# Unread products at the start, W1's raw copy in another place and its low parts on GpSimd, and a new order of the opening

## The chip, the cores and the metric

The kernel runs on one core of a Trainium2 chip. The metric is the device time of one execution in microseconds; a kernel's time is the median of its runs. Engines are named TensorE, VectorE, ScalarE, GpSimd and SyncE; in the rows they are PE (and PEld for its weight loads), DVE, ACT, POOL and SP, and a q behind a name is that engine's queue of transfers.

## What is computed

A linear attention with a decaying state, and two feed-forward stages behind it, all in float32. Batch 4, 8 heads, 768 tokens, head width 48; the model width is 8 x 48 = 384.

```python
for t in range(S):
    cur = einsum('bhd,bhe->bhde', u * k[t], v[t])
    y[t] = einsum('bhd,bhde->bhe', r[t], state + cur)
    state = w[t][..., None] * state + einsum('bhd,bhe->bhde', k[t], v[t])
h = y @ w_in                       # 3072 x 384 @ 384 x 1024
solu = h * softmax(h)
ln = (solu - mean(solu)) / sqrt(var(solu) + 1e-6) * g_ln
x2 = ln @ w_out                    # 1024 -> 384
g = maximum(0.01 * (x2 @ w_in2), x2 @ w_in2)     # 384 -> 2048
out = g @ w_out2                   # 2048 -> 384
```

## The kernel before

**Tiles.** The 768 tokens of each batch are cut into six chunks of 128. Three chunks make a super of 384 tokens. Attention and the first feed-forward stage up to the normalised rows go chunk by chunk; the matrix products behind them go super by super, 384 columns wide.

**A chunk.** Its decays are multiplied up by a scan (`decay`, L854), their inverse is taken (`inverse`, L864), the keys are divided by them (`undecayed_keys`, L869), GpSimd multiplies the queries by them (`decayed_queries`, L515) and ScalarE lays the queries of two heads side by side in `rb` (`part_heads`, L660). TensorE makes the scores (`scores`), VectorE masks them (`mask`, L877), GpSimd makes the keys as seen from the chunk's end (`end_keys`, L524), TensorE transposes these (`transpose_keys`, L1205) and ScalarE copies them out (`take_keys`, L682). `attend` makes the chunk's output, `fresh_state` its part of the state, `take_y` (L890) and `take_state` (L899 and L904) bring both back. ScalarE sums the decays and inverses for a later test of their range (`take_range`, L676). The output is transposed (`transpose_y`, L1198), copied to X (`take_x`, L667), multiplied with W1 (the expert product, 128 x 1024), its row maximum taken (`row_max`, L921), then the exponential (`exp_rows`, L643), the product with it (`times_exp`, L931), its statistics (`row_stats`, `row_moments`, L937 to L951), the row's scale on GpSimd (`row_scale`, L548 and L550) and the normalised rows (`normalise`, L650).

**Two ways of multiplying.** The steady part splits each weight and each moving operand into a high part, rounded to fp32r, and a low part, what is left, and uses three products (`HH`, `LH`, `HL`). ScalarE makes a weight's high part (`high_part`, L639) and VectorE the low one (`low_part`, L1014), both in groups of 768 columns: four for W1 and W2, eight for W3 and W4. The raw weight lies where the low part will be. The first three chunks can't wait for that, so they are multiplied in plain float32 out of the raw weights (two records in the trace for each product). For this reason `low_part(0, g)` waits until all six halves of the first expert products are done (`pe_h`), since it writes over what they read.

**The opening.** The first three chunks, with their loads, run in an order written out by hand for each engine. On SyncE: the loads of attention's inputs, the tokens, and W1 in two halves. On ScalarE: the heads, the range sums, the copies, the loads of W3 (`load_weights(2)`), W2 and W4, the high parts, and `take_ln` (L727), which multiplies transposed rows by the gain. On TensorE:

```python
pe.wait_ge(consts, 6)
first_scores(0); attend(0, 0, (0, 1)); first_keys(0); attend(0, 0, (2, 3)); first_state(0)
first_transposes(0); first_expert(0, (0,))
first_scores(1); first_keys(1); attend(0, 1); first_state(1)
first_scores(2); first_expert(0, (1,)); first_transposes(1); first_keys(2); attend(0, 2); first_state(2)
first_expert(1); first_transposes(2)
first_rows(0); first_expert(2); first_out(0)
```

and then `first_rows` (the transposes of normalised rows, L1324) and `first_out` (their product with W2) for the other two chunks. Each engine takes its instructions in this order, so what stands behind a waiting one waits too. The fourth chunk's decays, inverse, keys and heads are also made in the opening.

**Behind the opening** a list of steps (`batch_steps`) sets the order: each step makes one 128-row tile of a hidden layer for 384 tokens (`prod`), ScalarE and VectorE evict and split it, and TensorE adds its product with the second weight into the accumulators (`cons`). The next chunks' attention is spread over these steps in slots. The rest of W2's, W3's and W4's high and low parts is made in the first 16 steps (`LOW_PARTS`).

## Time and profile before

| | us |
|---|---|
| three runs | 793.64, 794.32, 795.70 |
| their median | 794.32 |
| the profiled execution | 793.65 |
| its span in the trace | 791.6 |
| TensorE busy in the span | 775.0 (98%) |
| VectorE busy | 520.8 (66%) |
| ScalarE busy | 341.1 (43%) |
| GpSimd busy | 173.2 (22%) |
| W3's transfer, from issue at 20.8 to landing | 15.4 |
| W4's transfer, from issue at 34.4 to landing | 15.6 |

The span runs from the first to the last instruction; the profiled execution's own time is 2.05 us longer. A busy share is an average over the whole span, in which the opening is less than a tenth. All times inside the trace count from the start of the span. The records of TensorE overlap, because one product's end lies over the next one's start; what a group of them takes is read from the timeline, and their pace is this time by their number.

### The profile page before, as it was taken

How to read it: one execution, taken by the hardware profiler on the slowest of the kernel's cores; microseconds unless marked ns; L12 is line 12 of the kernel's file. 1: busy time of each engine (PE TensorE's matmuls, PEld its weight loads, DVE VectorE, ACT ScalarE, POOL GpSimd, SP SyncE). 2: the span in 40 equal slices, each digit the busy share in tenths (PEclk: the TensorE clock that was granted, in tenths of full speed). 3: DMA queues.
4: the chain of work that ended last, by engine and by line, in shares of the span. 5: the costliest groups of instructions: out<-in, count | busy, mean ns of one | idle time of the engine just before them, and what ended most of it. 6: DMA issues, size and time to landing. Idle time of an engine off the chain costs nothing.

```text
span 791.6 us, 12116 instructions
## 1 busy us (share of the span) xinstructions
PE 775.0 (98%) x4624; PEld 735.3 (93%) x4624; DVE 520.8 (66%) x1023; ACT 341.1 (43%) x676; POOL 173.2 (22%) x199
## 2 busy tenths in 40 slices
PE   5999999999999999999999999999999999999997
PEld 4769999999999999999999999999999999999997
DVE  6788999966656666757757577485674766553332
ACT  3567554534344343443433444344343444334332
POOL 4514313221213202212212023022120221100000
PEclk9999999999999999999999999999999999999999
DMA  9940222022012021120220311202202110000001
GB/s 275 337 171 1 66 65 66 5 92 65 19 47 90 7 65 36 31 95 1 65 66 1 96 34 32 65 5 91 66 1 65 36 61 31 1 1 30 1 2 34
DMA packets 19666, 45.89 MB, mean 58 GB/s; under 512 B 1952, under 2 KB 14752, under 8 KB 19216
## 3 DMA queue, kind: packets, MB, share of 16 engines
q1 hardware_dynamic: 15952, 37.17, 15.4%
q10 hardware_dynamic: 3648, 7.87, 2.8%
q8 instruction: 39, 0.64, 0.3%
q14 instruction: 27, 0.22, 0.1%
HBM read 40.31 MB, written 4.72 MB: 57 GB/s over the span
## 4 chain that ended last, share of the span: by engine, by line
PE 79%; DVE 1%; issue 0%; ACT 0%; DVEq 0%
PE BANKS L1181 56%; PE MISC L1181 20%; PE BANKS L1360 2%; PE MISC L1205 1%; PE MISC L1198 1%; DVE ki L864 0%; DVE W2L L1014 0%; DVE att L854 0%; DVE A L877 0%; DVE Rraw L996 0%; DVE RL L1003 0%; DVE X2L L1020 0%; ACT X2H L734 0%; ACT OUT L740 0%; DVE diag L884 0%
## 5 line engine op out<-in xcount | busy, mean ns | idle before, releaser
L1181 PE MATMUL BANKS<-RH,W4H 128*128 128x384 f32 x384 | 135.5, 353 | 0.0
L1181 PE MATMUL BANKS<-X2H,W3H 128*128 128x384 f32 x384 | 130.7, 340 | 0.2 <-DVE X2L L1020 0.2
L1181 PE MATMUL BANKS<-X2L,W3H 128*128 128x384 f32 x384 | 129.3, 337 | 0.0
L1181 PE MATMUL BANKS<-X2H,W3L 128*128 128x384 f32 x384 | 129.2, 337 | 0.0
L1181 PE MATMUL BANKS<-RH,W4L 128*128 128x384 f32 x384 | 129.1, 336 | 0.0
L1181 PE MATMUL BANKS<-RL,W4H 128*128 128x384 f32 x384 | 129.0, 336 | 0.0
L996 DVE TENSOR_TENSOR Rraw<-BANKS,Rraw 128x384 f32<-128x384 f32 x128 | 70.7, 553 | 87.2 <-ACT Rraw L713 86.4
L713 ACT ACTIVATE Rraw<-BANKS 128x384 f32<-128x384 f32 x128 | 62.5, 488 | 137.0 <-PE BANKS L1181 136.7
L717 ACT ACTIVATE RH<-Rraw 128x384 fp32r<-128x384 f32 x128 | 67.1, 524 | 102.1 <-DVE Rraw L996 102.1
L864 DVE RECIPROCAL ki<-att 112x128 f32<-112x128 f32 x96 | 89.3, 937 | 0.0
L1003 DVE TENSOR_TENSOR RL<-Rraw,RH 128x384 fp32r<-128x384 f32 x128 | 71.1, 556 | 22.5 <-ACT RH L717 22.5
L1181 PEld LDWEIGHTS BANKS<-X2H,W3H 128*128 128x128 f32 x384 | 72.1, 188 | 0.6 <-issue 0.5
L1181 PEld LDWEIGHTS BANKS<-RH,W4L 128*128 128x128 f32 x384 | 72.4, 189 | 0.3
L1181 PEld LDWEIGHTS BANKS<-RH,W4H 128*128 128x128 f32 x384 | 72.3, 188 | 0.3
L1181 PEld LDWEIGHTS BANKS<-X2H,W3L 128*128 128x128 f32 x384 | 72.2, 188 | 0.1
L1181 PEld LDWEIGHTS BANKS<-X2L,W3H 128*128 128x128 f32 x384 | 72.1, 188 | 0.0
L1181 PEld LDWEIGHTS BANKS<-RL,W4H 128*128 128x128 f32 x384 | 72.1, 188 | 0.0
L524 POOL TENSOR_TENSOR ke<-att 112x512 f32<-112x512 f32 x20 | 22.6, 1132 | 217.8 <-ACT junk L676 163.7
L921 DVE TENSOR_REDUCE hmax<-MISC 128x1 f32<-128x512 f32 x44 | 30.2, 690 | 60.2 <-PE MISC L1181 60.1
L548 POOL TENSOR_TENSOR rstd<-vare,mhalf 128x1 f32<-128x1 f32 x24 | 14.8, 615 | 238.5 <-DVE vare L951 238.5
L1181 PE MATMUL BANKS<-RH,W2H 128*128 128x384 f32 x168 | 60.7, 361 | 0.0
L1005 DVE SCALAR_TENSOR_TENSOR RL<-BANKS,gain,RH 128x384 fp32r<-128x384 f32 x56 | 33.1, 591 | 41.3 <-ACT RH L719 41.3
(138 smaller groups left out, 1494.5 us busy)
## 6 DMA issues: line engine op xcount, KB each, us to landing
att<-rkw SPq DMA_DIRECT2D x23, 672.0 KB, 4.7
rtok<-r_tok SPq DMA_DIRECT2D x22, 192.0 KB, 2.5
ktok<-k_tok SPq DMA_DIRECT2D x22, 192.0 KB, 3.0
vtok<-v_tok SPq DMA_DIRECT2D x22, 192.0 KB, 4.0
out<-OUT SPq DMA_DIRECT2D x7, 576.0 KB, 4.3
W3raw<-w_in ACTq DMA_DIRECT2D x1, 3072.0 KB, 15.4
W4raw<-w_out ACTq DMA_DIRECT2D x1, 3072.0 KB, 15.6
W1raw<-w_in SPq DMA_DIRECT2D x2, 768.0 KB, 10.7
```

The costliest lines, as they stand in the source:

```text
L524: nc.gpsimd.tensor_tensor(ke(b, m)[:, :, :], keys(b, m), last, ALU.mult).then_inc(pool_ke, 1)
L548: nc.gpsimd.tensor_tensor(rstd[:, :], vare[:, :], mhalf[:, :], ALU.pow).then_inc(pool_rstd, 1)
L713: nc.scalar.activation(Rraw[:, fp % 3, :], PR[fp % 2][:, 0:ST], ACT.Copy, scale=0.01).then_inc(act_slope, 1)
L717: nc.scalar.activation(RH[:, fp % 3, :], Rraw[:, fp % 3, :], ACT.Copy).then_inc(act_hi, 1)
L864: nc.vector.reciprocal(ki[:, a, :], decays(b, m)[:, a, :]).then_inc(dve_inv, 1)
L921: nc.vector.reduce_max(hmax[:, n:n + 1], hidden(b, m)[:, n * 512:(n + 1) * 512], AX.X).then_inc(dve_max, 1)
L996: nc.vector.tensor_tensor(Rraw[:, fp % 3, :], PR[fp % 2][:, 0:ST], Rraw[:, fp % 3, :], ALU.max).then_inc(dve_relu, 1)
L1003: nc.vector.tensor_tensor(RL[:, fp % 3, :], Rraw[:, fp % 3, :], hi, ALU.subtract).then_inc(dve_lo, 1)
L1005: nc.vector.scalar_tensor_tensor(RL[:, fp % 3, :], PR[fp % 2][:, 0:ST], gain[:, f:f + 1], hi, ALU.mult, ALU.subtract).then_inc(dve_lo, 1)
L1181: return nc.tensor.matmul(dst, lhsT, rhs, start=start, stop=stop, skip_group_check=True)
L1198: last = nc.tensor.transpose(XT[:, k * CH:(k + 1) * CH], tokens(0, b, m)[:, k * 128:(k + 1) * 128], ident[:, :])
L1360: last = nc.tensor.transpose(dst[:, c * CH:(c + 1) * CH], LN[:, c, f * 128:(f + 1) * 128], ident[:, :])
```

## The change

It does six things.

1. **Unread products.** VectorE first fills 128 columns of `EXP` with ones. TensorE makes four products of these columns by themselves, 512 columns wide, before its first wait for the constants, then one between the scores of pairs 0, 1 and those of pairs 2, 3, one behind these, and one behind the first chunk's state. They go to the first accumulator bank and nobody reads them.
2. **W1's raw copy** lies in the space of W2's high part and no longer in that of W1's low part. The low parts then have nothing to wait for but their high parts.
3. **W1's low parts on GpSimd**, two ahead of the first row scale and two ahead of the second; VectorE's four are gone. W1's four high parts on ScalarE come sooner, behind the third chunk's range sums.
4. **Rows scaled sooner.** On VectorE the first chunk's product with the exponential, its statistics and moments come ahead of the third chunk's `take_y` and `take_state`. On ScalarE `normalise(0, 0)` comes right behind its `exp_rows`. GpSimd makes the second and third row scales between the steps of the fourth chunk.
5. **The fourth chunk's decays** and first two inverses come ahead of the second chunk's row maximum on VectorE, its other inverses between the third chunk's steps; its heads on ScalarE come behind the last gain pass, its range sums ahead of it.
6. **W4's load** comes behind the first normalisation, and the high parts of W3 and W4 take new places.

```diff
-        W1raw = sb("W1raw", [128, KM * FF1], F32, over="W1L")
+        W1raw = sb("W1raw", [128, KM * FF1], F32, over="W2H")
...
+            def low_part(g):
+
+                pool.wait_ge(split_hi[0], g + 1)
+                nc.gpsimd.tensor_tensor(group(W1L, 0, g), group(W1raw, 0, g), group(W1H, 0, g).bitcast(F32),
+                                        ALU.subtract).then_inc(split_lo[0], 1)
...
             own_token(0, 2, 1)
+            for g in range(2):
+                low_part(g)
             row_scale(0, 0)
-            row_scale(0, 1)
-            row_scale(0, 2)
             decayed_queries(0, 3)
             decayed_state(0, 3)
+            for g in range(2, 4):
+                low_part(g)
+            row_scale(0, 1)
             own_token(0, 3, 0)
+            row_scale(0, 2)
             end_keys(0, 3)
...
             load_weights(1)
             part_heads(0, 2)
             take_range(0, 2)
+            for g in range(4):
+                high_part(0, g)
             take_x(0, 1)
             take_keys(0, 2)
+            exp_rows(0, 0)
+            normalise(0, 0)
             load_weights(3)
-            exp_rows(0, 0)
-            for g in range(2):
-                high_part(2, g)
-            for g in range(3):
-                high_part(0, g)
+            high_part(2, 0)
             take_x(0, 2)
-            normalise(0, 0)
             exp_rows(0, 1)
             take_ln(0)
-            for g in range(2, 4):
+            for g in range(1, 3):
                 high_part(2, g)
             normalise(0, 1)
-            high_part(0, 3)
             exp_rows(0, 2)
+            take_ln(1)
+            high_part(2, 3)
+            normalise(0, 2)
+            take_range(0, 3)
+            take_ln(2)
+            part_heads(0, 3)
+            high_part(3, 0)
+            high_part(3, 1)
             for g in range(4, 6):
                 high_part(2, g)
-            take_ln(1)
-            high_part(3, 0)
-            normalise(0, 2)
-            part_heads(0, 3)
-            high_part(3, 1)
-            take_ln(2)
-            take_range(0, 3)
             take_x2(0, 0)
...
             def low_part(w, g):
                 dve.wait_ge(split_hi[w], g + 1)
-                if w == 0:
-                    dve.wait_ge(pe_h, 2 * CPS)
...
+            nc.vector.memset(EXP[:, 0:128], 1.0).then_inc(filled, 1)
...
             row_max(0, 0)
-            take_y(0, 2)
-            take_state(0, 2)
             times_exp(0, 0)
             row_stats(0, 0)
             row_moments(0, 0)
+            take_y(0, 2)
+            take_state(0, 2)
+            decay(0, 3)
+            for a in (0, 1):
+                inverse(0, 3, a)
+            row_max(0, 1)
             low_part(2, 0)
-            row_max(0, 1)
-            low_part(2, 1)
             times_exp(0, 1)
             row_stats(0, 1)
             row_moments(0, 1)
+            low_part(2, 1)
             row_max(0, 2)
-            for g in range(2, 4):
-                low_part(2, g)
+            inverse(0, 3, 2)
             times_exp(0, 2)
             row_stats(0, 2)
             row_moments(0, 2)
-            low_part(0, 0)
-            decay(0, 3)
-            for a in range(PAIRS):
-                inverse(0, 3, a)
-            low_part(0, 1)
+            inverse(0, 3, 3)
             undecayed_keys(0, 3)
-            low_part(0, 2)
+            for g in range(2, 4):
+                low_part(2, g)
             low_part(3, 0)
-            low_part(0, 3)
...
+            def unread(n):
+                for i in range(n):
+                    mm(ACC[0], EXP[:, 0:128], EXP[:, 0:128].unsqueeze(1).broadcast_to([128, 4, 128]), True, True)
+
+            pe.wait_ge(filled, 1)
+            unread(4)
             pe.wait_ge(consts, 6)
-            first_scores(0)
+            scores(0, 0, (0, 1))
+            unread(1)
+            scores(0, 0, (2, 3))
+            unread(1)
             attend(0, 0, (0, 1))
             first_keys(0)
             attend(0, 0, (2, 3))
             first_state(0)
+            unread(1)
             first_transposes(0)
```

## Rows read from the trace of the kernel before

**Rows 1.** Stretches: start:end, length, then busy us and count per engine, clock, DMA.

```profile
7.72:18.30 10.58, 10.48 (x39) 8.45 (x39) 7.78 (x15) 2.71 (x7) 5.04 (x5) 1.00 1.05 305
23.45:43.36 19.91, 19.91 (x113) 14.70 (x111) 14.62 (x31) 9.01 (x16) 9.49 (x11) 1.00 1.03 350
43.36:45.07 1.71, 0.00 (x1) 0.00 (x0) 1.67 (x4) 1.67 (x3) 0.11 (x1) 1.00 1.06 372
45.07:71.78 26.71, 26.45 (x193) 22.89 (x193) 23.93 (x47) 20.92 (x48) 8.10 (x9) 1.00 0.14 50
100.00:785.00 685.00, 684.06 (x4099) 659.11 (x4099) 439.30 (x869) 284.44 (x561) 134.66 (x148) 1.00 0.14 42
```

**Rows 2.** Timeline of TensorE: start, duration, what, and idle time before it.

```profile
7.72 4.20 PE L1181 MATMUL MISC<-rb,att 112*128 112x256 f32 x8 [7.72 <-ACT rb L660]
...
18.87 4.74 PE L1181 MATMUL BANKS<-W1raw,X 128*128 128x512 f32 x6 [0.58 <-ACT X L667]
23.45 1.89 PE L1181 MATMUL BANKS<-rb,att 112*128 112x256 f32 x8
25.18 0.55 PE L1205 MATMUL MISC<-ident,first_ke 112*128 112x112 f32 x4
...
26.44 1.91 PE L1181 MATMUL MISC<-tok,A 128*128 128x48 f32 x16
28.18 0.99 PE L1181 MATMUL MISC<-tok,keT 128*112 128x96 f32 x8
...
30.95 2.74 PE L1181 MATMUL BANKS<-W1raw,X 128*128 128x512 f32 x6
...
45.07 0.66 PE L1324 MATMUL BANKS<-ident,LN 128*128 128x128 f32 x4 [1.71 <-ACT LN L650]
```

**Rows 3.** Timeline of VectorE; last, the keys' line over 0 to 80 (min/median/max ns).

```profile
9.37 0.42 DVE L869 TENSOR_TENSOR att<-att,ki 112x256 f32<-112x256 f32 x1
...
10.98 0.67 DVE L877 TENSOR_TENSOR A<-MISC,causal 128x512 f32<-128x512 f32 x1
12.04 0.69 DVE L877 TENSOR_TENSOR A<-MISC,causal 128x512 f32<-128x512 f32 x1 [0.39 <-PE MISC L1181]
...
16.11 0.56 DVE L890 TENSOR_TENSOR rtok<-MISC,rtok 128x384 f32<-128x384 f32 x1 [1.26 <-PE MISC L1181]
...
20.63 1.35 DVE L854 TENSOR_TENSOR_SCAN att<-att,BANKS 112x128 f32<-112x128 f32 x4
21.89 1.74 DVE L864 RECIPROCAL ki<-att 112x128 f32<-112x128 f32 x2
...
38.55 1.28 DVE L931 TENSOR_TENSOR EXP<-BANKS,EXP 128x512 f32<-128x512 f32 x2
...
L869 DVE TENSOR_TENSOR att<-att,ki x5: 425/692/1484, 7.1 to 63.5; 112x512 f32<-112x512 f32 x3, 112x256 f32<-112x256 f32 x2
```

**Rows 4.** Timeline of ScalarE.

```profile
29.58 0.19 ACT L676 ACTIVATION_READ_ACCUMULATOR junk<-att 112x1 f32 x1
34.05 0.49 ACT L667 ACTIVATE X<-MISC 128x384 f32<-128x384 f32 x1 [4.29 <-PE MISC L1198]
...
37.72 2.29 ACT L639 ACTIVATE W1H<-W1raw 128x768 fp32r<-128x768 f32 x3
...
43.79 1.23 ACT L650 ACTIVATE LN<-EXP,nbias,rstd 128x1024 f32<-128x1024 f32 x1
...
69.49 1.25 ACT L734 ACTIVATE X2H<-BANKS 128x384 fp32r<-128x384 f32 x3 [2.16 <-PE BANKS L1181]
```

**Rows 5.** GpSimd: line L537 over 0 to 80, and two rows of its timeline.

```profile
L537 POOL TENSOR_TENSOR rtok<-rtok,ktok x2: 995/1344/1692, 12.0 to 62.7; 128x384 f32<-128x384 f32 x2
```
...
32.45 0.83 POOL L540 TENSOR_TENSOR tok<-tok,diag 128x384 f32<-128x384 f32 x1 [0.75 <-DVE diag L884]
...
42.01 1.20 POOL L548 TENSOR_TENSOR rstd<-vare,mhalf 128x1 f32<-128x1 f32 x1 [8.72 <-DVE vare L951]
```

**Rows 6.** Landing of the fourth chunk's attention inputs, issued at 30.2 (L411).

```profile
DMA to landing us min/median/max: 8.4/8.4/8.4
```

More of the change, by code:

```diff
@@ L255, in build @@
         consts, chain = sem("consts"), sem("chain")
-        ld_decay, ld_w1a = sem("ld_decay"), sem("ld_w1a")
+        ld_decay, ld_w1a, filled = sem("ld_decay"), sem("ld_w1a"), sem("filled")
         split_hi = [sem(f"split_hi{i}") for i in range(4)]
@@ L1259, in fresh_state, with scores @@
                 last.then_inc(pe_state, 1)
-            def scores(b, m):
+            def scores(b, m, pairs=range(PAIRS)):
                 if first(b, m - 1) and not first(b, m):
@@ L1266, in scores @@
                     wait(pe, act_keT, chunks(b, m, 1, 1))
-                for a in range(PAIRS):
+                for a in pairs:
                     if first(b, m):
```

## The prediction

> **What bounds the kernel now.** I read the stretches first, then TensorE in order of time, then the engines that release it. After 71.78 us TensorE is the bound: from 100 to 785 it is busy 684.06 of 685.00 us [rows 1], so nothing that another engine gains there shortens the run. The change can gain only in the opening, before TensorE's dense work begins, and each microsecond by which the opening ends sooner should come off the span one for one. The reader is to see three things there. TensorE has nothing to do until 7.72 [rows 2]. Then its products run at half pace: 8 records of scores take 4.20 at 7.72 but 1.89 at 23.45, and 6 records of the expert product take 4.74 at 18.87 but 2.74 at 30.95 [rows 2]. Last, it stands idle for 1.71, from 43.36 to 45.07, waiting for ScalarE's normalised rows [rows 1, 2]. The column of the granted clock says 1.00 in every stretch [rows 1], so here it is the durations that show the level: a factor of 2.2 for one and the same product reads as 1.2 GHz until late in the first expert product and 2.4 GHz after.
>
> **The change, part by part.**
>
> *Unread products at the start.* VectorE fills 128 columns at about 1 us and TensorE begins on four 128x512 products, two records each. By the 6 records at each level [rows 2] a record costs 4.74 / 6 = 0.79 or 2.74 / 6 = 0.46, so the four cost between 8 x 0.46 = 3.7 and 8 x 0.79 = 6.3 us and end between 5 and 7.6 if they begin at 1.3. The scores become ready at 7.72, so they should be delayed by 0, at worst by 0.3. The question is whether this stretch lifts the clock. Before, it rose while TensorE ran 512-column products without a pause (18.87 to 23.45), and had not risen in the mostly narrow work ahead of them. The four unread products are work of the former kind, and more of it than stood there before the rise, so I take it that the level is 2.4 GHz when the scores start. The bounds are: at 7.72 (value taken), or not before the expert product, as now.
>
> *Stage A, 7.72 to the second chunk's scores (23.45 now), at the high pace.* The work is summed by rows at that pace. Scores of pairs 0 and 1 take half of 1.89, to 8.7; an unread product of 0.9 to 9.6. Pairs 2 and 3 need VectorE's keys, which end at 9.37 + 0.42 = 9.8 [rows 3], so they end at 10.75. The second unread product fills to 11.65, where the first mask ends anyway (10.98 + 0.67 [rows 3]). First half of attention: half of the 16 records' 1.91 [rows 2], to 12.6. VectorE's second mask loses its wait of 0.39 [rows 3] and ends near 12.3, in time. Key transposes 0.55 [rows 2] to 13.1, second half of attention to 14.1, state 0.99 [rows 2] to 15.1. The third unread product stands ahead of the transposes and costs its 0.9 in full, to 16.0, less what TensorE would have waited: VectorE's sum (0.56) can't start before 14.5, where its own earlier work ends (16.11 less the idle 1.26 and the 0.39 [rows 3]), and ends at 15.1. Transposes 0.5, ScalarE's copy 0.5: the expert product starts at 17.0 and, at 2.74, ends at 19.7. Second scores at 19.7 against 23.45: **-3.75 us**. VectorE follows: with its 0.39 and 1.26 of waiting gone, its keys for the second chunk, ready when the next scan starts at 20.63 [rows 3], are ready at 19.0; 19.7 is not gated by them.
>
> *Stage B, 23.45 to 43.36.* TensorE is busy 19.91 of 19.91 us, at high pace [rows 1]. Same products, so 0 if the feeders move along by 3.75. VectorE does, within 0.3. ScalarE gets the four high parts of W1 here, 4 x 0.76 (three take 2.29 [rows 4]) = 3.1 us. They start after the range sums, which end at 29.77 now [rows 4] and near 26.5 then (VectorE's 3.3 sooner), and so end near 29.6; the copy of X behind them starts at 34.05 now [rows 4], 30.3 then. They are covered, by 0.7 us. Without that cover the delay would reach TensorE's third expert product only after the 5 us of its second.
>
> *Stage C, the normalised rows.* ScalarE's exponential follows X and keT: 34.05 + 0.83 now, 31.1 then, plus 1.3 = 32.4. VectorE's product starts at 38.55 now because the sum and the state of the third chunk, which wait on TensorE, stand ahead of it [rows 3]; the change puts them behind, so it starts at 32.4. From there to GpSimd is 42.01 - 38.55 = 3.46, GpSimd and its hand-over 43.79 - 42.01 = 1.78 and the normalisation 1.23 [rows 4, 5]: 38.9. TensorE asks for it at 43.36 - 3.75 = 39.6. The wait of 1.71 goes: **-1.71 us**. What was waited for next is ScalarE's copy of X for the third expert product: it stands behind one high part of W3 and ends near 40.3, while TensorE is at its eight transposes until 40.6. W4's load, moved behind the normalisation, starts near 39 instead of 34.4; its first use moves later than 58, so its price is 0.
>
> *GpSimd's low parts.* No row has this operation there. By a 128x384 operation, 995 ns at least and 1692 ns at worst beside VectorE [rows 5], a 128x768 one costs 2.0 to 3.4 us. I take 2.0, since VectorE reads PSUM in much of that time. Two of them stand ahead of the first row scale: GpSimd is free at 32.45 + 0.83 - 3.75 = 29.5 [rows 5], so they end between 33.5 and 36.3; the row scale is wanted at 32.4 + 3.46 = 35.9. At the upper end 0.4 is lost, inside the 0.7 of slack. The second two stand between the decays and the second row scale, 41 to 45 or 48; this scale is wanted at 46.2 and TensorE wants its rows at 51, 2 us after they come even at the upper end. On VectorE four operations go; since it isn't the path there, that is slack only.
>
> What those rows show of sharing is that VectorE's product of two SBUF operands took 1484 ns where the median was 692, beside GpSimd's 1692 for 995 [rows 3, 5]. The Trainium skill (SBUF — State Buffer, the section on the engine side's shared port pair) says that GpSimd and a two-port VectorE operation exclude each other, so that the loser fully blocks. It speaks against this part; by it a low part could last the length of whatever VectorE runs besides its own, which the traced worst case of 1.7 times already prices, so the sum stays as it is.
>
> *The fourth chunk's decays, sooner on VectorE.* Scans 1.35 and two reciprocals 1.74 [rows 3] now stand ahead of the second chunk's row maximum. The maximum's input, TensorE's second expert product, is ready near 39.2 (its y transposes follow and end at 43.36 - 3.75 = 39.6); VectorE gets there at 35.9 + 1.2 (sum and state) + 3.1 = 40.2: 1.0 late. Behind it, in order: maximum 1.4, ScalarE's exponential 1.3, its gain pass (first part at 43.3). TensorE wants that at 40.6 + twice 2.6 = 45.8, after the third expert product, so the 1.0 is hidden in 2.5 us. The scan also needs the fourth chunk's transfer: it landed 8.4 us after its issue at 30.2 [rows 6]; issued near 27 it lands at 35.3, wanted at 37.
>
> *Stage D, 45.07 to 71.78.* 26.45 of 26.71 busy [rows 1]: 0. ScalarE's order is tighter at the end: heads and four high parts (1.3 + 3.3) less the range sums (1.5) stand ahead of the copies to X2H, which begin at 69.49 now after an idle 2.16 [rows 4]. Shifted by 5.45 they would begin at 64.1; they begin at 65.2. VectorE's part ends 1 us later, at 66.2, and TensorE, after its fourth scores, asks at 66.3. Hidden by 0.1, so up to 0.5 could be lost; I put 0.15.
>
> **Sum:** -3.75 - 1.71 + 0.15 = -5.3 us. The profiled execution took 793.65, so it gives 788.35. The median of the three runs lies 0.67 above the profiled one, and the forecast for a median is 794.32 - 5.3 = **789.0**. (Under 0.3%, 2.4 us, a measurement of this kernel can't be told from no change.)
>
> **Rivals.**
> 1. *Clock falls back in the short work.* TensorE is idle from 5-7.6 to 7.7 and has only narrow products from 11.65 to 15.1. For: narrow work did not lift the clock before. Against: from 25 to 29 us narrow work of the same kind ran at high pace [rows 2], and so did what followed 1.71 us of idleness. If it falls only around 16, the expert product costs 4.74: start 17.0, end 21.7, -1.75 - 1.71 = -3.5: 790.8. If it falls already at 11.7, attention begins as now and the third unread product adds 1.6: +1.6 - 1.7 = 0: 794.2.
> 2. *The rows still come late.* Some of VectorE's or GpSimd's chain slips (low parts at 3.4 us or more, the fourth chunk's transfer late) and up to 1.7 of stage C returns: -3.7: 790.6.
> 3. *Slower: the clock doesn't rise before the scores.* Place: the three unread products between scores, attention and transposes. Each then costs 2 x 0.79 = 1.6 on a path on which TensorE is already busy 10.48 of 10.58 us [rows 1]: +4.8, and 0.2 at the start, less the 1.71: +3.2: 797.5. It decides if the first four products don't lift the clock; against it stands that a shorter run of wide products did so later in this trace.
>
> The Trainium skill (TensorE: Matmul & The Clock Gate, "What's actually happening") has the default state as throttled and activity as what releases it. By that the forecast holds; no row here shows it from the very start of a kernel.
>
> **Chances.** Forecast 0.62 (its own range 787.7 to 790.2), rival 1's milder form 0.10, rival 2 0.13, rival 1's harder form 0.09, rival 3 0.06. The first three are faster: 0.85. Same 0.09, slower 0.06. The range reaches from -6.8 (stage D's and B's small waits vanish as well, and a copy chain half a microsecond shorter) to the milder rivals with half a microsecond on top: 787.5 to 791.8.
>
> **What would show it.** Right: unread records about 0.8 us apart first and 0.45 at the end; the first 8 score records at the pace of the 1.89 us row and not of the 4.20 one; the expert product's 6 records in 2.7 us from about 17; second scores near 19.7; no idleness between the third chunk's transposes of y and the transposes of rows; the first dense product near 66.4 instead of 71.78. Wrong: score records at the pace of the 4.20 row (rival 3); the expert product again at 4.7 us (rival 1); an idle gap on TensorE released by ScalarE's rows or copies between 38 and 47 (rival 2); any idleness after 66 us that TensorE doesn't have now.

## The result, and the profile after

The changed kernel took 788.33 us in the median of five runs (788.04 to 792.25), the kernel before 795.32 in the median of five beside it. The ratio is 0.9938, with a 95% interval of 0.9915 to 0.9961: faster by 0.6%, some 4.9 us. The two plain medians lie 7.0 apart, but the kernel before stood at 793.6 to 794.2 in the four later groups of runs, so the smaller figure is used. On a second chip (the first experiment) it came to 0.9943 (0.9924 to 0.9962), 4.5 us. The forecast was 789.0, in a range of 787.5 to 791.8: both the direction and the size came out.

Of the changed kernel there are two profiled executions, and they differ. The first took 792.25 with a span of 790.1, the second 788.53 with a span of 786.4. The second stands for most runs, so it is read first. TensorE in order of time (start, duration, what, and idle time before it):

```profile
1.13 6.07 PE L1187 MATMUL BANKS<-EXP 128*128 128x512 f32 x8 [1.13 <-DVE EXP L1080]
7.84 1.10 PE L1187 MATMUL MISC<-rb,att 112*128 112x256 f32 x4 [0.63 <-DVE att L878]
...
15.04 1.05 PE L1187 MATMUL BANKS<-EXP 128*128 128x512 f32 x2
...
17.34 2.84 PE L1187 MATMUL BANKS<-W1raw,X 128*128 128x512 f32 x6 [0.58 <-ACT X L677]
20.02 1.89 PE L1187 MATMUL BANKS<-rb,att 112*128 112x256 f32 x8
...
26.66 1.97 PE L1187 MATMUL BANKS<-rb,att 112*128 112x256 f32 x8 [0.92 <-issue]
28.46 2.74 PE L1187 MATMUL BANKS<-W1raw,X 128*128 128x512 f32 x6
...
40.39 0.49 PE L1204 MATMUL MISC<-ident,tok 128*128 128x128 f32 x3
40.72 0.60 PE L1330 MATMUL BANKS<-ident,LN 128*128 128x128 f32 x4
...
67.36 0.42 PE L1187 MATMUL BANKS<-X2H,W3H 128*128 128x384 f32 x1
```

Against [rows 2]: the first scores run at once at the pace of the later ones, the first expert product takes 2.84 and not 4.74, the second chunk's scores start at 20.02 instead of 23.45, the transposes of rows at 40.72 instead of 45.07, without a wait. The first dense product starts at 67.36; it was 71.78, the end of a stretch in [rows 1]. One thing is new: a pause of 0.92 ahead of the third chunk's scores at 26.66. "issue" there names no releaser, but VectorE's keys of that chunk end just before it, at 25.38 + 1.18 = 26.56:

```profile
25.38 1.18 DVE L878 TENSOR_TENSOR att<-att,ki 112x512 f32<-112x512 f32 x1
```

The other engines in the same execution, ScalarE first, then GpSimd:

```profile
37.94 1.24 ACT L660 ACTIVATE LN<-EXP,nbias,rstd 128x1024 f32<-128x1024 f32 x1 [4.34 <-POOL nbias L556]
39.08 0.83 ACT L649 ACTIVATE W3H<-W3raw 128x768 fp32r<-128x768 f32 x1
```

```profile
41.57 4.31 POOL L548 TENSOR_TENSOR W1L<-W1raw,W1H 128x768 fp32r<-128x768 f32 x2
L548 POOL TENSOR_TENSOR W1L<-W1raw,W1H x2: 1812/2176/2541, 41.6 to 43.3; 128x768 fp32r<-128x768 f32 x2
...
47.56 1.20 POOL L554 TENSOR_TENSOR rstd<-vare,mhalf 128x1 f32<-128x1 f32 x1 [1.67 <-DVE vare L960]
```

The normalised rows are done at 39.18 (37.94 + 1.24), 1.5 us ahead of TensorE, and wait for GpSimd's scale alone; in [rows 4] they were done at 45.02 (43.79 + 1.23). Of GpSimd's second two low parts the first takes 1.81 and the other 2.54 (the second line gives shortest, mean and longest in ns); both are done 1.67 us before VectorE's next moments.

In the first execution, the one of 792.25, the same places look so:

```profile
20.03 1.89 PE L1187 MATMUL BANKS<-rb,att 112*128 112x256 f32 x8
...
26.68 3.59 PE L1187 MATMUL BANKS<-rb,att 112*128 112x256 f32 x8 [0.92 <-issue]
30.06 2.84 PE L1187 MATMUL BANKS<-W1raw,X 128*128 128x512 f32 x6
...
49.02 5.62 PE L1187 MATMUL BANKS<-OUT,W2raw 128*128 128x128 f32 x48 [0.42 <-DVE LN L940]
...
69.78 0.42 PE L1187 MATMUL BANKS<-X2H,W3H 128*128 128x384 f32 x1
```

Behind the pause the scores take 3.59 us, not 1.97. The granted clock of that stretch, the third column from the end (start:end, length, busy and count, clock, share and rate of transfers), tells why:

```profile
23.00:26.60 3.60, 2.76 (x26) 1.00 1.02 270
26.60:30.00 3.40, 3.32 (x8) 0.54 1.00 344
```

It fell from 2.4 to 1.2 GHz for about that stretch, after narrow products and a pause. Later VectorE stood 1.78 us for the fourth chunk's inputs:

```profile
41.61 1.37 DVE L863 TENSOR_TENSOR_SCAN att<-att,floor 112x128 f32<-112x128 f32 x4 [1.78 <-DMA att<-rkw]
```

Their transfer landed 13.9 us after its issue at 27.7, where it had taken 8.4 [rows 6]; in the second execution it took 10.2. The two together put the dense part 2.42 us later (69.78 against 67.36). The two executions lie 3.7 apart; the other 1.3 come behind TensorE's last product, which is taken up below.

### The profile page after: what moved, and what is told of

Its sections match the earlier page's. It is cut to its first block, busy times and chain, and to the rows that moved or that the text cites. A ratio compares the mean times of both kernels' runs of the same rounds, so it can differ in the third digit from the quotient of the medians.

```text
span 790.1 us, 12141 instructions
## 1 busy us (share of the span) xinstructions
PE 779.6 (99%) x4638; PEld 735.4 (93%) x4638; DVE 517.6 (66%) x1020; ACT 341.5 (43%) x676; POOL 179.5 (23%) x203
## 4 chain that ended last, share of the span: by engine, by line
PE 80%; DVE 1%; issue 0%; ACT 0%; DVEq 0%
PE BANKS L1187 56%; PE MISC L1187 20%; PE BANKS L1366 2%; PE MISC L1211 1%; PE MISC L1204 1%; DVE ki L873 0%; DVE W2L L1021 0%; DVE att L863 0%; DVE A L886 0%; DVE Rraw L1005 0%; DVE RL L1012 0%; DVE X2L L1027 0%; ACT X2H L744 0%; ACT OUT L750 0%; DVE diag L893 0%
## 5 line engine op out<-in xcount | busy, mean ns | idle before, releaser
L1187 PE MATMUL BANKS<-RH,W4H 128*128 128x384 f32 x384 | 135.4, 353 | 0.0
L1187 PE MATMUL BANKS<-X2H,W3H 128*128 128x384 f32 x384 | 130.8, 341 | 0.2 <-DVE X2L L1027 0.2
L1187 PE MATMUL BANKS<-X2L,W3H 128*128 128x384 f32 x384 | 129.4, 337 | 0.0
L1187 PE MATMUL BANKS<-RH,W4L 128*128 128x384 f32 x384 | 129.2, 336 | 0.0
L1187 PE MATMUL BANKS<-X2H,W3L 128*128 128x384 f32 x384 | 129.2, 336 | 0.0
L1187 PE MATMUL BANKS<-RL,W4H 128*128 128x384 f32 x384 | 129.0, 336 | 0.0
L727 ACT ACTIVATE RH<-Rraw 128x384 fp32r<-128x384 f32 x128 | 67.1, 524 | 101.5 <-DVE Rraw L1005 101.5
L1187 PEld LDWEIGHTS BANKS<-X2H,W3H 128*128 128x128 f32 x384 | 72.1, 188 | 0.6 <-issue 0.5
L1187 PEld LDWEIGHTS BANKS<-RH,W4L 128*128 128x128 f32 x384 | 72.4, 188 | 0.3
L1187 PEld LDWEIGHTS BANKS<-RH,W4H 128*128 128x128 f32 x384 | 72.2, 188 | 0.3
L1187 PEld LDWEIGHTS BANKS<-X2H,W3L 128*128 128x128 f32 x384 | 72.1, 188 | 0.1
L1187 PEld LDWEIGHTS BANKS<-RL,W4H 128*128 128x128 f32 x384 | 72.1, 188 | 0.0
L1187 PEld LDWEIGHTS BANKS<-X2L,W3H 128*128 128x128 f32 x384 | 72.1, 188 | 0.0
L554 POOL TENSOR_TENSOR rstd<-vare,mhalf 128x1 f32<-128x1 f32 x24 | 14.1, 589 | 225.3 <-DVE vare L960 225.3
L1187 PE MATMUL BANKS<-RH,W2H 128*128 128x384 f32 x168 | 60.6, 361 | 0.0
```

What stands on the lines that cost most here:

```text
L554: nc.gpsimd.tensor_tensor(rstd[:, :], vare[:, :], mhalf[:, :], ALU.pow).then_inc(pool_rstd, 1)
L727: nc.scalar.activation(RH[:, fp % 3, :], Rraw[:, fp % 3, :], ACT.Copy).then_inc(act_hi, 1)
L1187: return nc.tensor.matmul(dst, lhsT, rhs, start=start, stop=stop, skip_group_check=True)
```

## The experiments

Each was timed in five rounds, beside runs of the kernel before on the same chip; their median lay between 793.63 and 794.21 in all four groups of runs, so ratios are compared. A profile shows one execution, and often not the median one.

**The changed kernel again.** No edit.

> The changed kernel once more, for the spread and for a second profile. In the first profile of it the scores of the third chunk took 3.59 us (1.89 to 1.97 elsewhere) after a pause of 0.92, and the execution took 792.25 where four others took 788.0 to 789.7. Theory A (the clock falls in some executions only, and that is the 3 to 4 us between them): an execution near 788 has these scores at 1.9 to 2.0 us and its first dense product near 66 to 67 instead of 69.78. Theory B (the pause and the half pace are there each time, and what differs lies elsewhere): 3.59 again also at 788.

Measured: 789.04, six runs from 786.98 to 791.73. The profile is the one shown first. Theory A: the pause is there in both profiles, the half pace behind it is not. The mean granted clock of a whole run fits this: the two runs above 790 have 0.998 and 0.996, the others 0.999 or 1.0.

**The unread products alone, in the kernel before.**

```diff
+            nc.vector.memset(EXP[:, 0:128], 1.0).then_inc(filled, 1)
...
+            unread(4)
             pe.wait_ge(consts, 6)
-            first_scores(0)
+            scores(0, 0, (0, 1))
+            unread(1)
+            scores(0, 0, (2, 3))
+            unread(1)
...
             first_state(0)
+            unread(1)
```

> The kernel before with the unread products alone. Theory A (the early pace is worth its 3.75 us by itself, because TensorE is the path from 18 to 43 us): 3.5 to 4 us faster than before, the idle 1.7 us ahead of the transposes of rows still there. Theory B (VectorE and the transfers hold the early work back, so the pace is worth nothing without the new order): under 1.5 us faster, with new idle stretches on TensorE before 43.

Measured: 793.35, ratio 1.0000 (0.9986 to 1.0014). No gain at all, which theory B had, though its reason was only half right. TensorE first, then ScalarE:

```profile
19.63 1.89 PE L1182 MATMUL BANKS<-rb,att 112*128 112x256 f32 x8
...
39.99 0.49 PE L1199 MATMUL MISC<-ident,tok 128*128 128x128 f32 x3
44.53 1.11 PE L1325 MATMUL BANKS<-ident,LN 128*128 128x128 f32 x4 [4.06 <-ACT LN L650]
45.44 1.06 PE L1325 MATMUL MISC<-ident,LN 128*128 128x128 f32 x4
46.29 6.85 PE L1182 MATMUL MISC<-W1raw,X 128*128 128x512 f32 x12
```

```profile
39.20 1.58 ACT L639 ACTIVATE W3H<-W3raw 128x768 fp32r<-128x768 f32 x2 [4.07 <-DMA W3raw<-w_in]
40.68 2.29 ACT L639 ACTIVATE W1H<-W1raw 128x768 fp32r<-128x768 f32 x3
42.88 0.47 ACT L667 ACTIVATE X<-MISC 128x384 f32<-128x384 f32 x1
43.25 1.23 ACT L650 ACTIVATE LN<-EXP,nbias,rstd 128x1024 f32<-128x1024 f32 x1
```

TensorE is 3.8 us ahead at the second scores and still 2.9 ahead at 39.99, and then waits 4.06 for the rows. The rows wait in ScalarE's order behind W3's high parts, and those for W3's transfer. This took 20.3 us where it had taken 15.4: issued 1.9 sooner, it landed 3.0 later, at 39.2. The transfers are saturated all the time (share 1.03 in [rows 1]), and W2's load now follows 3.1 behind W3's. In the eleven profiles where it does, W3's takes 17.5 to 20.5; in the three where W2's follows 4.6 to 5.3 behind, 14.8 to 15.6. That W2's load is what delays it was not tested. Behind the wait the next product begins at half pace (6.85 for the 5.32 it takes elsewhere), and the dense part starts at 73.61, 1.8 later than before. All of the early gain is lost between 40 and 53. This was one of the longest of the twelve executions, 795.93; the shortest, 791.27 with a mean clock of 1.0, shows that the loss isn't always as large.

**The changed kernel without its unread products.**

```diff
-            unread(4)
...
-            unread(1)
...
-            unread(1)
...
-            unread(1)
```

> The changed kernel without its seven unread products. Theory A: only the idle 1.71 us ahead of the transposes of rows is gained, 1.5 to 2 us faster than before, the first scores at 4.2 us. Theory B (the new order carries most of the gain): 4 us or more faster than before.

Measured: 791.39, ratio 0.9971 (0.9960 to 0.9981), 2.3 us faster than before. Theory A. First scores 4.26, second scores at 23.46 as before, transposes of rows at 43.22 without a wait; the first dense product at 69.87. So the new order alone is worth 2.3 us, the unread products alone nothing, and both together 4.5 to 4.9.

**Only the four ahead of the scores.** The three later ones are taken out of the changed kernel.

> The changed kernel with the four unread products ahead of the scores, but not the three later ones. Theory A (the four raise the clock and it stays up, the three are only in the way): 0.5 to 0.9 us faster than the changed kernel, since the one ahead of the transposes goes. Theory B (the three keep the clock up through the narrow work): attention or the first expert product falls to half pace (4.7 us) and it is 1.5 to 3 us slower than the changed kernel.

Measured: 791.02, ratio 0.9968 (0.9954 to 0.9982), no better than without any. Theory B. The dense part starts at 69.79, without any at 69.87. TensorE:

```profile
7.92 1.10 PE L1187 MATMUL MISC<-rb,att 112*128 112x256 f32 x4 [0.73 <-DVE att L878]
10.10 1.13 PE L1187 MATMUL MISC<-rb,att 112*128 112x256 f32 x4 [1.08 <-DVE att L878]
12.04 1.29 PE L1187 MATMUL MISC<-vtok,A 128*128 128x48 f32 x8 [0.81 <-DVE A L886]
...
13.90 1.81 PE L1187 MATMUL MISC<-vtok,A 128*128 128x48 f32 x8
...
18.50 5.05 PE L1187 MATMUL BANKS<-W1raw,X 128*128 128x512 f32 x6 [0.58 <-ACT X L677]
```

The clock is high at the scores and falls during the first half of attention, after three waits: granted 0.56 of full from 12 to 18. In all but one of twelve runs the mean clock is 0.995 or lower, which no other kernel's median run shows.

**Only the three later ones.**

```diff
-            pe.wait_ge(filled, 1)
-            unread(4)
```

> The changed kernel without the four unread products ahead of the scores, but with the three later ones: the case of the prediction's slower rival, in which the three are paid at half pace. Theory A (the four are what lifts the clock): the scores take 4.2 us, the unread products 1.6 each, the second chunk's scores start at 26 to 28 instead of 20, and the kernel is 3 to 5 us slower than the one without any unread product (791.4), that is 794.5 to 796.5. Theory B (the scores with the unread products between them are wide work enough and lift the clock by themselves within the first chunk): the third unread product and the first expert product run at 0.9 and 2.8 us, and it is within 1 us of the kernel without any.

Measured: 790.08 (788.45 to 790.38, five runs), ratio 0.9949 (0.9936 to 0.9963). Theory A fell:

```profile
7.64 2.05 PE L1187 MATMUL MISC<-rb,att 112*128 112x256 f32 x4 [7.64 <-ACT rb L670]
9.48 1.91 PE L1187 MATMUL BANKS<-EXP 128*128 128x512 f32 x2
11.19 1.39 PE L1187 MATMUL MISC<-rb,att 112*128 112x256 f32 x4
12.42 1.02 PE L1187 MATMUL BANKS<-EXP 128*128 128x512 f32 x2
...
20.81 1.89 PE L1187 MATMUL BANKS<-rb,att 112*128 112x256 f32 x8
```

The clock rises within the second half of the scores, at about 12 us. The second scores start at 20.81, only 0.8 later than with all seven, and the dense part at 67.67, only 0.3 later. By theory B it would be within 1 us of the kernel without any; it is 1.3 faster by the medians, 1.7 by the ratios. So the three products between the narrow ones carry the gain on TensorE, and the four in the idle time ahead of them add little: 0.3 in these two profiles, and nothing that the intervals of the ratios could show. Which of the three is needed was not tested.

**The third chunk's sum and state first on VectorE again.**

```diff
-            times_exp(0, 0)
-            row_stats(0, 0)
-            row_moments(0, 0)
             take_y(0, 2)
             take_state(0, 2)
+            times_exp(0, 0)
+            row_stats(0, 0)
+            row_moments(0, 0)
```

> The changed kernel with the third chunk's sum and state back ahead of the first chunk's product with the exponential on VectorE. Theory A (VectorE's order is what removed the wait ahead of the transposes of rows): that product starts 2 to 2.5 us later, the transposes wait 1.5 to 2 us again, and the kernel is 1.5 to 3.5 us slower than the changed one (3.5 if the clock falls behind the wait). Theory B (it was ScalarE's order, with W3's high parts out of the way): within 0.7 us of the changed kernel.

Measured: 789.88 (789.56 to 792.83), ratio 0.9955 (0.9937 to 0.9972), about 1 us slower than the changed kernel by the ratios, which their intervals don't separate. In its profile the product with the exponential starts at 35.96, not 33.63; TensorE waits 0.79 for the rows and 1.48 ahead of its first product with W2, the latter because the fourth chunk's inputs land at 42.1 there (VectorE idle 2.83). That is a late landing, 14.5 us after the issue, as in the first execution of the changed kernel (13.9), and not the price of this order. The wait for rows was expected at 1.5 to 2. The wait is 4.06 with the old order on both engines and 0.79 with the new one on all but VectorE, so ScalarE's order, which has no transfer ahead of the rows any more, is the larger part of what removed it.

**A part of ScalarE's order, beside the unread products in the kernel before.** Two high parts of W3 go behind the first normalisation, nothing else moves.

```diff
             exp_rows(0, 0)
-            for g in range(2):
-                high_part(2, g)
             for g in range(3):
                 high_part(0, g)
             take_x(0, 2)
             normalise(0, 0)
+            for g in range(2):
+                high_part(2, g)
             exp_rows(0, 1)
```

> The kernel before with the unread products, and on ScalarE the first two high parts of W3 behind the first normalisation instead of ahead of it; nothing else. Unread products alone gained nothing: ScalarE stood 4.07 us for W3's transfer, ahead of the normalisation, TensorE then stood 4.06 us, and its next product ran at half pace (6.85 instead of 5.32 us). Theory A (that transfer, whose landing does not move with TensorE, is what held the gain back): the wait for it leaves TensorE's path, idle 2 us or less, 2 to 4 us faster than before. Theory B (VectorE's order holds it back as well): idle 3 us or more still, under 1 us faster.

Measured: 792.50, ratio 0.9989 (0.9975 to 1.0002). Between the two theories: the wait for the rows falls from 4.06 to 1.71, as theory A had it, but TensorE gets two new ones:

```profile
42.58 0.66 PE L1325 MATMUL BANKS<-ident,LN 128*128 128x128 f32 x4 [1.71 <-ACT LN L650]
...
56.10 5.62 PE L1182 MATMUL BANKS<-OUT,W2raw 128*128 128x128 f32 x48 [1.05 <-ACT OUT L727]
...
63.95 5.60 PE L1182 MATMUL BANKS<-OUT,W2raw 128*128 128x128 f32 x48 [1.35 <-ACT OUT L727]
```

The dense part starts at 71.51, only 0.3 sooner than before. Both new waits are for ScalarE's gain passes, so the rest of the old order is then the limit: a part of the new order moves the wait along.

**W1's low parts on VectorE again**, its raw copy again in W1L's space.

```diff
-        W1raw = sb("W1raw", [128, KM * FF1], F32, over="W2H")
+        W1raw = sb("W1raw", [128, KM * FF1], F32, over="W1L")
...
-            for g in range(2):
-                low_part(g)
             row_scale(0, 0)
...
-            for g in range(2, 4):
-                low_part(g)
             row_scale(0, 1)
...
+                if w == 0:
+                    dve.wait_ge(pe_h, 2 * CPS)
...
             for g in range(2, 4):
                 low_part(2, g)
+            for g in range(4):
+                low_part(0, g)
             low_part(3, 0)
```

> The changed kernel with W1's raw copy and its low parts back where they were: in W1L's space, on VectorE, ahead of W4's first low part. Theory A (the move to GpSimd is slack only): within 0.7 us of the changed kernel, since VectorE idles 4.25 us near 62 in it. Theory B (VectorE's four operations would hold back the copies for the dense part): 1 us or more slower, with an idle stretch on TensorE between 62 and 72.

Measured: 788.04 (786.95 to 788.95, six runs, none above 789), ratio 0.9922 (0.9904 to 0.9939). Theory A: the raw copy's new place and the move to GpSimd bring nothing, and what difference there is speaks against them. The intervals don't show that it is faster. Its dense part starts at 66.83, 0.53 sooner than in the second execution, but so do its second scores (19.49 for 20.02), which the edit doesn't touch.

**The second half of the expert product ahead of the third scores.**

```diff
-            first_scores(2)
             first_expert(0, (1,))
+            first_scores(2)
```

> The changed kernel with the second half of the first expert product ahead of the third chunk's scores on TensorE. In both profiles of the changed kernel TensorE stood 0.92 us before these scores, and in the slower one it ran at half pace behind that. Theory A (the pause costs its 0.9 and, in some executions, the clock): 0.7 to 1.5 us faster than the changed kernel, no idle stretch between 20 and 38, and less spread between executions. Theory B (the row chain of chunk 0 or the masks of chunk 2 become the limit when the scores come 1.8 us later): same or slower, with a new wait near 32 or 40.

Measured: 789.33, ratio 0.9949 (0.9927 to 0.9970). The profiled execution is the fastest of all, 786.64, with the dense part from 66.14 and no pause at 26. But the twelve runs reach from there to 796.51 (mean clock 0.995). Its second scores, ahead of the edit, already start 0.51 sooner (19.51), so the swap is worth 0.7 of the 1.22 us at the dense part. What comes behind TensorE's last product is 1.2 us or more shorter than in most profiles, and the edit doesn't touch that either: the 786.64 is in part luck. The pause can be worked away, but neither theory fits: the median doesn't show the gain, and the spread didn't shrink. One run has 793.63 at a mean clock of 0.999, so the clock isn't all that differs between executions.

**One more unread product in the pause**, into the second bank.

```diff
-            def unread(n):
+            def unread(n, bank=0):
                 for i in range(n):
-                    mm(ACC[0], EXP[:, 0:128], EXP[:, 0:128].unsqueeze(1).broadcast_to([128, 4, 128]), True, True)
+                    mm(ACC[bank], EXP[:, 0:128], EXP[:, 0:128].unsqueeze(1).broadcast_to([128, 4, 128]), True, True)
...
+            unread(1, 1)
             first_scores(2)
```

> The changed kernel with one more unread product, into the second accumulator bank, where TensorE stood 0.92 us ahead of the third chunk's scores. It moves nothing forward: its 0.9 us fill the pause. Theory A (the pause is what lets the clock fall in some executions): the median stays within 0.7 us of the changed kernel's, the execution stretch above 790 is gone or rarer (three of eleven executions of the changed kernel were above 790). Theory B (what differs between executions lies elsewhere, in landings of transfers and the last store): the same share above 790.

Measured: 788.75, ratio 0.9944 (0.9925 to 0.9962). Three of twelve runs are above 790, of the changed kernel it was three of eleven, and two (793.23 and 794.90) have a mean clock of 0.997. The share above 790 is as large as before, which theory B had; but the two long ones show a lower clock, so with the pause filled the clock still falls in some executions. Where it falls in those isn't known, since none of them was the profiled one.

**The second chunk's row maximum ahead of the fourth chunk's decays.**

```diff
+            row_max(0, 1)
             decay(0, 3)
             for a in (0, 1):
                 inverse(0, 3, a)
-            row_max(0, 1)
             low_part(2, 0)
```

> The changed kernel with the second chunk's row maximum back ahead of the fourth chunk's decays on VectorE. In the slower of its two profiles VectorE stood 1.78 us for the fourth chunk's transfer, which landed 13.9 us after its issue, and TensorE then 0.42 us for VectorE ahead of its first product with W2; in the other, the transfer landed in time. Theory A (this order costs only when that transfer is late): within 0.7 us of the changed kernel's median, with fewer long executions. Theory B (the decays must come early, or the fourth chunk is late for the dense part): a new idle stretch on TensorE behind 60 and 0.7 us or more slower.

Measured: 792.37, ratio 0.9974 (0.9959 to 0.9990): 2.5 us or more slower than the changed kernel. Neither theory had its cause. First VectorE, then GpSimd, then TensorE:

```profile
43.52 3.22 DVE L1021 TENSOR_TENSOR W3L<-W3raw,W3H 128x768 fp32r<-128x768 f32 x1
46.66 1.27 DVE L940 TENSOR_TENSOR LN<-BANKS,LN 128x512 f32<-128x512 f32 x2
...
49.93 0.95 DVE L1021 TENSOR_TENSOR W3L<-W3raw,W3H 128x768 fp32r<-128x768 f32 x1
```

```profile
43.32 0.83 POOL L530 TENSOR_TENSOR fresh<-state,att 112x384 f32<-112x384 f32 x1
44.11 4.29 POOL L548 TENSOR_TENSOR W1L<-W1raw,W1H 128x768 fp32r<-128x768 f32 x2
L548 POOL TENSOR_TENSOR W1L<-W1raw,W1H x2: 1809/2163/2517, 44.1 to 45.9; 128x768 fp32r<-128x768 f32 x2
```

```profile
47.99 7.25 PE L1187 MATMUL BANKS<-OUT,W2raw 128*128 128x128 f32 x48 [1.94 <-DVE LN L940]
```

One low part of W3 lasts 3.22 us on VectorE, 0.95 when it is alone. It begins inside GpSimd's state (43.32 to 44.15) and goes on through the whole of GpSimd's first low part of W1 (1.81, to 45.92). It ends at 46.74, 0.82 behind that, which is nearly the length of one alone; GpSimd's second low part lasts 2.52 in turn. TensorE waits 1.94 behind it and then runs at half pace for a while (7.25 for 5.52). The Trainium skill (SBUF — State Buffer, the section on the engine side's shared port pair) has a VectorE operation with two inputs in SBUF and a GpSimd operation that reads SBUF excluding each other, the loser blocked for the whole instruction; these rows agree. In the changed kernel VectorE's operation begins 0.8 us behind the start of GpSimd's (41.57 in the second execution), not 0.6 ahead of it:

```profile
42.37 1.83 DVE L1021 TENSOR_TENSOR W3L<-W3raw,W3H 128x768 fp32r<-128x768 f32 x1
```

It ends at 44.20, again 0.82 behind GpSimd's first low part (41.57 + 1.81 = 43.38), and its slack covers this.

**All that spoke for itself together**: the swap on TensorE, the low parts on VectorE and the row maximum first.

> What the runs so far speak for, together: the changed kernel with the second half of the first expert product ahead of the third chunk's scores, W1's low parts on VectorE again, and the second chunk's row maximum ahead of the fourth chunk's decays. Theory A (the three are independent): 0.5 to 1.5 us faster than the changed kernel, first dense product near 66. Theory B (GpSimd's low parts and the new place of the decays hid something): same or slower than the changed kernel, with idle stretches on TensorE that its profile shows.

Measured: 788.44 (787.05 to 793.15, six runs), ratio 0.9939 (0.9914 to 0.9963): the same as the changed kernel. Its dense part starts at 66.17, where theory A had it; the gain in time didn't come. GpSimd, then VectorE:

```profile
42.57 1.79 POOL L530 TENSOR_TENSOR fresh<-state,att 112x384 f32<-112x384 f32 x1
```

```profile
42.78 0.89 DVE L1019 TENSOR_TENSOR W3L<-W3raw,W3H 128x768 fp32r<-128x768 f32 x1
```

W3's low part meets GpSimd's state again, 0.2 behind its start as in the run before, but it takes 0.89, and it is GpSimd's that is stretched, 1.79 for 0.83. So the rows show that one of the two stands, and not which. With GpSimd's low parts gone the row maximum ahead of the decays costs TensorE nothing, which confirms the cause in the run before. A version that measurably beats the changed kernel wasn't found; the low parts on VectorE alone have the lowest ratio.

## Why the prediction was right, and where it was not

**Direction and size: right, with some luck.** -5.3 was forecast; the ratios give -4.9 and -4.5. The opening of the second execution ends 71.78 - 67.36 = 4.42 sooner, that of the first only 2.00. The second one's span is shorter by 5.2 (791.6 - 786.4). Its dense part took 0.4 longer, which no step had, and the other 1.2 lie behind TensorE's last product, before and in the second execution:

```profile
785.92 0.33 PE L1181 MATMUL BANKS<-RL,W4H 128*128 128x384 f32 x1
```

```profile
781.90 0.33 PE L1187 MATMUL BANKS<-RL,W4H 128*128 128x384 f32 x1
```

From its end to the end of the span it is 5.3 us before and 4.2 here, but 5.5 in the first execution. Over all fourteen profiles it is 3.9 to 4.2 in five and 5.2 to 5.7 in nine, whatever the edit. No step of the change touches that, so of the agreement to 0.1 us in the second span 0.8 is luck.

**Stage A: right.** Second scores at 20.02 for 19.7, -3.43 for -3.75. The 0.3 goes with a landing: the u vector took 8.1 us (7.0 before), GpSimd stood 0.83 for it and VectorE 0.65 for GpSimd in turn. In the six profiles with all unread products where it took 6.5 to 7.7, the second scores start at 19.4 to 19.6; in the four where it took 8.1 or 8.2, at 19.9 to 20.2. The third unread product stood in the path as forecast (15.04, transposes at 16.2), but by the runs with only four and only three it belongs to those that hold the clock, so it can't be booked as a price alone.

**The unread products: right that they act, wrong which of them.** The prediction gave the work to the four in the idle time and called the later three filler on two waits and a cost on the third. The runs show the reverse: four alone lose the clock in attention and bring nothing, three alone raise it and come within 0.3 us at the dense part.

**Stage B: wrong by 0.95.** "So 0 if the feeders move along by 3.75. VectorE does, within 0.3." It doesn't: its keys for the third chunk are ready at 26.56, TensorE wants them at 25.7. They came 2.49 sooner than before (29.05), TensorE 3.43. VectorE has hardly an idle moment from 16 to 26.6, so what it can gain there is the idle time it had, and its product of two SBUF operands took 1.18 beside GpSimd where 0.69 is usual [rows 3]. This is the step that failed: the slack of VectorE was not summed up to this point.

**Stage C: right.** Product at 33.63 for 32.4, rows ready at 39.2 for 38.9, asked for at 40.7 for 39.6, no wait. But the step named VectorE's order as what brings it; the run that undoes VectorE's order and the one that makes a part of ScalarE's alone show that taking W3's transfer out from ahead of the rows does at least as much. That transfer wasn't costed: at TensorE's new pace it would have been late by 4 us. The fourth chunk's transfer was, and by the same error: forecast to land at 35.3 and wanted at 37, it landed at 37.9 in one execution and at 41.6 in the other.

**Stage D: right.** The copies to X2H were forecast to hold by 0.1; 67.36 follows the transposes of rows by 26.64, before it was 26.71.

**GpSimd's low parts: the price right, its reach too short.** 1.8 us each were measured for the first two, 1.8 and 2.5 for the others, where 2.0 was taken from 2.0 to 3.4. But 1.7 times was a bound for GpSimd's own operation. What a low part does to VectorE's beside it was not priced: 1.9 times in the changed kernel (1.83 for 0.95), 3.4 times with the row maximum first.

**Rivals.** Rival 1 happened, in some executions: at 26.7, not at 11.7 or 16, and with only the four ahead at 12. Rival 2 happened in the same execution by the fourth chunk's transfer, for 0.42. Rival 3 was set up by the three later products alone and gave 790.1, not 797.5: the scores with the unread products among them lifted the clock by themselves.

## What to carry to other kernels

When a gain in one engine's pace moves everything forward, list what doesn't move: transfers on saturated queues, and engines with little idle time up to that point. Two parts of a change can be worth less apart (0 and 2.3 us here) than together (4.5 to 4.9). Work without a reader paid here between the narrow products that stand in the path, and not in the idle time ahead of them; in another kernel, test both places apart, and each product by itself, which was not done here. And before a single profile is read for its span, look at what differs ahead of the edit and behind the last product.

## What the runs showed of the hardware

The column of the granted clock stays at 1.00 before the first rise, although the products run at half pace there; after the first rise it tells a fall, 0.54 of full in the stretch of 3.4 us shown above. The first eight unread records took 5.25 to 6.61 us in the profiles that have them, from the same start at 1.13, so the rise came at differing times. A fall can follow a wait of 4.06 us, of 1.94, or several under 1.1 with narrow products around them; after one and the same pause of 0.92 it came in one profile and not in another, and it did not come after 1.71 [rows 1] or 1.48 (the run with the third chunk's sum first). A VectorE product of two SBUF operands and GpSimd's operation beside it stretch one another: 3.22 and 1.83 for 0.95 on VectorE, 1.79 for 0.83 on GpSimd. And the same kernel's landings of a 672 KB transfer, issued at the same time, differed by 3.7 us (13.9 and 10.2).
